# Attention with hashed buckets and two gated layers: sign sums in two PSUM banks, turning of the next pair moved behind other work

## What is computed

```python
# q, k, v: (2, 8, 768, 64)  proj: (64, 6)
q_bits = (einsum('bhsd,dk->bhsk', q, proj) > 0)          # 6 signs per row
k_bits = (einsum('bhsd,dk->bhsk', k, proj) > 0)
mask = (q_bucket[..., :, None] == k_bucket[..., None, :])  # buckets: the 6 signs read as a number
scores = where(mask, scale * q @ k.T, -1e9)
attn = exp(scores - max); attn /= sum(attn) + 1e-9
x = attn @ v                       # (1536, 512) after the heads are joined
x = (sigmoid(x @ w_gate) * (x @ w_val)) @ w_out            # 512 -> 1536 -> 512
h = x @ w_in; x = hinge(h) @ w_out2                        # 512 -> 2048 -> 512
```

## Time and profile before

| | us |
|---|---|
| median of 3 runs | 788.66 (788.01 to 789.24) |
| the profiled execution | 787.32 |
| its span | 785.2 |
| PE busy in the span | 772.7 (98%) |
| DVE, ACT, POOL busy | 557.0, 461.1, 539.0 |

### The profile page before, as it was taken

How to read it: one execution, slowest core, us unless ns; L and a number is a source line. 1 busy time by engine, 2 the same in 40 slices (tenths; PEclk the granted TensorE clock), 3 DMA queues, 4 the chain that set the end, 5 groups by cost and what they waited for, 6 DMA issues and landing times.

```text
span 785.2 us, 12182 instructions
## 1 busy us (share of the span) xinstructions
PE 772.7 (98%) x4403; PEld 716.2 (91%) x4403; DVE 557.0 (71%) x862; ACT 461.1 (59%) x731; POOL 539.0 (69%) x533
## 2 busy tenths in 40 slices
PE   7999999999999999999999999999999999999998
PEld 6999999999989999999899999999899988999996
DVE  6888888888888656565864666676777676756654
ACT  4888988988997443344453333357455465644433
POOL 4667667788889987877596977746957755565420
PEclk9999999999999999999999999999999999999999
DMA  6896586385100222122021211120121111201002
GB/s 153 182 194 135 133 176 132 80 168 131 55 1 1 81 81 81 31 77 81 28 82 55 81 54 53 55 81 28 59 77 55 36 45 45 91 27 54 1 1 80
DMA packets 61930, 60.08 MB, mean 77 GB/s; under 512 B 28384, under 2 KB 51632, under 8 KB 61872
## 3 DMA queue, kind: packets, MB, share of 16 engines
q1 hardware_dynamic: 61712, 59.32, 29.5%
q10 hardware_dynamic: 160, 0.00, 0.0%
HBM read 37.75 MB, written 3.15 MB: 52 GB/s over the span
## 4 chain that ended last, share of the span: by engine, by line
PE 81%; ACT 6%; DVE 5%; issue 4%; POOL 3%; DMA 0%; SPq 0%; POOLq 0%; DVEq 0%; ACTq 0%
PE ps L758 12%; PE ps L759 12%; PE ps L760 12%; PE ps L787 9%; PE ps L799 6%; PE ps L800 6%; PE ps L798 5%; PE ps L788 4%; PE ps L724 4%; ACT ph L916 3%; PE ps L741 2%; PE ps L742 2%; DVE probs L1209 2%; PE ps L712 2%; PE ps L715 2%
## 5 line engine op out<-in xcount | busy, mean ns | idle before, releaser
L758 PE MATMUL ps<-xop,wset 128*128 128x384 f32 x560 | 190.7, 341 | 1.6 <-DVE u L1284 1.4
L759 PE MATMUL ps<-xop,wset 128*128 128x384 f32 x560 | 189.2, 338 | 0.0
L760 PE MATMUL ps<-xop,wset 128*128 128x384 f32 x560 | 188.8, 337 | 0.0
L1284 DVE TENSOR_TENSOR u<-ps,u 128x384 f32<-128x384 f32 x144 | 79.5, 552 | 103.4 <-PE ps L760 102.8
L526 POOL TENSOR_TENSOR wset<-stage,wset 128x512 fp32r<-128x512 f32 x39 | 58.1, 1490 | 108.5 <-ACT wset L963 108.5
L758 PEld LDWEIGHTS ps<-xop,wset 128*128 128x128 f32 x560 | 105.1, 188 | 14.4 <-issue 2.8
L1220 DVE TENSOR_TENSOR pl<-ps,ph 128x768 fp32r<-128x768 f32 x96 | 91.4, 954 | 26.6 <-ACT ph L916 25.7
L759 PEld LDWEIGHTS ps<-xop,wset 128*128 128x128 f32 x560 | 105.3, 188 | 3.5
L501 POOL TENSOR_SCALAR probs<-probs,small 128x768 f32<-128x768 f32 x96 | 88.3, 927 | 24.9 <-DVE small L1214 22.1
L760 PEld LDWEIGHTS ps<-xop,wset 128*128 128x128 f32 x560 | 105.2, 188 | 0.0
L532 POOL TENSOR_TENSOR wset<-wsum,wset 128x1024 fp32r<-128x1024 f32 x39 | 95.2, 2442 | 0.0
(11 more groups left out here) (134 smaller groups left out, 1685.8 us busy)
## 6 DMA issues: line engine op xcount, KB each, us to landing
stage<-in_moe_w_in_dram SPq DMA_DIRECT2D x16, 512.0 KB, 3.4
stage<-in_moe_w_out_dram SPq DMA_DIRECT2D x14, 512.0 KB, 3.8
stage<-in_moe_w_gate_dram SPq DMA_DIRECT2D x12, 512.0 KB, 4.2
stage<-in_moe_w_val_dram SPq DMA_DIRECT2D x12, 512.0 KB, 3.6
ops<-qh SPq DMA_DIRECT2D x15, 384.0 KB, 5.2
ops<-kh SPq DMA_DIRECT2D x28, 192.0 KB, 5.2
qn<-in_q_dram SPq DMA_DIRECT2D x16, 192.0 KB, 4.4
kn<-in_k_dram SPq DMA_DIRECT2D x16, 192.0 KB, 5.3
```

The costliest lines, as they stand in the source:

```text
L758: pe.matmul(dst, high[:, c, :], high_x(r)[:, c, :], start=(c == 0), stop=False)
L759: pe.matmul(dst, high[:, c, :], low_x(r)[:, c, :], start=False, stop=False)
L760: last = pe.matmul(dst, low[:, c, :], high_x(r)[:, c, :], start=False, stop=(c == 1))
```

## The change

The sign sums of q and k of the next pair go to two banks: of q to bank 7, of k to bank 6 (in pair 0's own sums both stay in bank 7). Each is a closed group of six matmuls with its own signal, and each has its own bits, made by an instruction of 64 rows instead of one of 128 for both. The signs of k wait for one more `o_copied`, and the weighings that take bank 7 and bank 6 next wait for the bits of q and of k. All pairs have one timetable: q turned at u = 1 and k at u = 4, signs at u = 3 and u = 6, bits ahead of `evacuate` at u = 4 and u = 7. On TensorE `turn` stands behind the weighing of its step, not ahead of it, and on ScalarE `high_turned` stands behind `exponential`, not ahead of it. The list `uses` follows: Q now stands behind the S and T of u = 1, K behind those of u = 4.

```diff
-        def late(i):
-            return 0 if i else 2
+        TURN = {"Q": 1, "K": 4}
+        SIGNS = {"Q": 3, "K": 6}
+        BITS = {"Q": 4, "K": 7}
...
-            if late(g // U) <= g % U < late(g // U) + 2 and g // U < NP - 1:
-                uses.append(("QK"[g % U - late(g // U)], g // U + 1))
+            for kind in "QK":
+                if g % U == TURN[kind] and g // U < NP - 1:
+                    uses.append((kind, g // U + 1))
...
-        z_bank = ps[:, 7, 0:G]
+        def z_bank(i, keys):
+            return ps[:, 6 if keys and i else 7, 0:G]
+        def bits_made(i, keys):
+            return 2 * i + keys if i else 1
...
-                if u == late(i) + 5 and i < NP - 1:
+                if u == BITS["K"] and i < NP - 1:
                     scale_codes(i + 1)
...
-                if i > 1 and not keys:
-                    pe.wait_ge(o_copied, 4 * (i - 1) - 2)
+                if i > 1:
+                    pe.wait_ge(o_copied, 4 * (i - 1) - (2 - keys))
...
-                        pe.wait_ge(z_bits, 2)
-                    if j % 4 == 3:
-                        pe.wait_ge(z_bits, min((j + 1) // 4 + 2, NP))
+                        pe.wait_ge(z_bits, bits_made(1, False))
+                    if j % 4 == 3 and j // 4 + 2 < NP:
+                        pe.wait_ge(z_bits, bits_made(j // 4 + 2, False))
+                    if j % 4 == 0 and j // 4 + 1 < NP:
+                        pe.wait_ge(z_bits, bits_made(j // 4 + 1, True))
...
-                if u == late(i) and i < NP - 1:
-                    turn("Q", i + 1)
-                if u == late(i) + 1 and i < NP - 1:
-                    turn("K", i + 1)
                 j, part = divmod(g - 8, HT)
                 if j >= 0:
                     weigh(j, part)
-                if u == late(i) + 3 and i < NP - 1:
+                if u == TURN["Q"] and i < NP - 1:
+                    turn("Q", i + 1)
+                if u == TURN["K"] and i < NP - 1:
+                    turn("K", i + 1)
+                if u == SIGNS["Q"] and i < NP - 1:
                     signs(i + 1, False)
-                if u == late(i) + 4 and i < NP - 1:
+                if u == SIGNS["K"] and i < NP - 1:
                     signs(i + 1, True)
...
-                if u == late(i) and i < NP - 1:
+                exponential(g)
+                if u == TURN["Q"] and i < NP - 1:
                     high_turned("Q", i + 1)
-                if u == late(i) + 1 and i < NP - 1:
+                if u == TURN["K"] and i < NP - 1:
                     high_turned("K", i + 1)
-                exponential(g)
...
-                if u == late(i) + 5 and i < NP - 1:
-                    make_bits(i + 1)
+                if u == BITS["Q"] and i < NP - 1:
+                    make_bits(i + 1, False)
+                if u == BITS["K"] and i < NP - 1:
+                    make_bits(i + 1, True)
                 evacuate(g)
```

## The result

The changed kernel takes 796.59 us (795.37 to 799.92, four runs) against 788.61: 1.0107 times as long, interval 1.0091 to 1.0122. The forecast was 795.5, slower. The profiled execution took 795.37 us against 787.32.

A forecast was written before the change was run, and what follows sets the result against it. TensorE was taken to bound the kernel. Pair 0 (+3.2 us) and pairs 1 to 6 (+3.6) gave 6.8 on 787.3, 794.1; the median lies 1.3 above, so 795.5, with an 8-in-10 range of 791 to 799.5.

The forecast's parts named there:

- What bounds the kernel: TensorE, nearly always busy in attention and layers, so attention's gain or loss moves the end one for one.
- Two banks: Second bits instruction on VectorE, 0.6 us in each of seven pairs, hidden behind TensorE; freeing the bank sooner wins nothing: 0.
- the walk: Step-by-step start times for pair 3 and pair 0, built from measured distances between instructions; pair 3 becomes 0.6 us longer.
- Removed stalls: Waits of q at u = 0 and k at u = 1 go: 0.7 us in each of six pairs.
- The new stalls: Scores of u = 3 and 6 wait for low parts of q and k: +3.6 us over pairs 1 to 6.
- the bounds 0 to 1.0: Extra time per steady pair: even if step-to-step edges are 0.1 us shorter, 1.0 us if ScalarE lags more.
- its sign: What the trace after should show: a pair of 29.4 to 29.9 us where it was 29.03.
- Pair 0: First pair, where `evacuate` of u = 2 now stands behind the low part of q: +3.2 us, between +2.0 and +3.6.
- SP's queue: Copies of k and the codes are issued later but still land in time for the next pair: 0.
- the stalls only trade places: Rival: edges are shorter, steady pairs stay even and only pair 0 loses: 791 us, chance 0.13.
- The faster one: Rival: 0.7 us gained in seven pairs because VectorE and ScalarE are never late: 784 us, chance 0.08.
- The growing lag: Rival: ScalarE enters u = 1 later by 0.3 or 0.4 us, 1.0 us or more per pair: 798 to 800, chance 0.12.

The follow-up runs named there:

- e3: The kernel before with two banks alone, turning at its old steps and in its old order: 787.90 us, ratio 0.9998.
- e10: e6 with q's bits of pair 0 at u = 7, not 6: 786.53 us, ratio 0.9982 to the kernel before.
- e5: The changed kernel with idle transposes filling TensorE's idle time in pair 0: 795.80 us, ratio 1.0099 to the kernel before.
- e8: The changed kernel with the second copy of a finished half head ahead of the exponential at u = 2 and 5: 794.03 us.
- e2: The changed kernel with turning ahead of the weighing and high part ahead of the exponential again, timetable and banks kept: 786.59 us, ratio 0.9980.
- e7: The changed kernel with turning ahead of the weighing again, the high part still behind the exponential: 796.18 us, ratio 1.0106 to the kernel before.
- e1: The changed kernel with the high part ahead of the exponential again, turning still behind the weighing: 793.97 us, ratio 1.0067 to the kernel before.
- e9: e1 with the second copy of a finished half head ahead of the exponential at u = 2 and 5: 791.61 us, ratio 1.0046.
- e6: e2 with the old steps of turning, signs and bits in pair 0: 786.26 us, ratio 0.9976 to the kernel before.

## Why the prediction was right
The forecast was 795.5 with 6.8 us of loss; 8.05 us were measured on the profiled executions (787.32 to 795.37) and 8.0 on the medians. In the trace pair 0 lost 3.4 us where 3.2 was said and pairs 1 to 6 lost 5.4 where 3.6 was said; the last pair, which has nothing to turn and no term in the forecast, gained 0.5. So nearly all of the miss is in the steady pairs, and the last pair made good 0.5 us of it by luck.

- *What bounds the kernel.* Right: the layers start 8.4 us later and end 8.4 us later.
- *Two banks.* Forecast 0, e3 measured 0.9998. That VectorE's second bits instruction lies in TensorE's shadow is right for the later pairs; in pair 0 it costs 0.8 us (e10), which the walk of pair 0 had among its steps. The bits of 64 rows take 0.60 to 0.62 us, the whole price of 128 rows, as taken.
- *Removed stalls.* Right: steps 0 and 1 at 2.07 and 2.63 us.
- *The new stalls.* The mechanism was right link by link. Forecast for the scores of u = 3, 4, 6 and 7 of pair 3, counted from the pair's start: 7.36, 10.71, 15.66 and 19.0 us; measured 7.21, 10.72, 15.85 and 19.41. So q's part was right to 0.15 us, k's was too small by 0.4. Two links were left out of the walk. At u = 4 ScalarE makes the high part of the turned probabilities ahead of the exponential, so that the exponential starts at 111.43 and not at 111.07, 0.99 us behind `evacuate` (110.08). And the signs of k do wait for the copy, by 0.18 us, where I had found the two even. The pair is 0.9 us longer, within the bounds 0 to 1.0 but not 0.6, and at 29.96 just above the 29.4 to 29.9 that were named as its sign. The six pairs took 179.5 us and 174.1 before, 5.4 longer, within 0 to +6.
- *Pair 0.* Forecast +3.2, measured +3.4. The walk gave 20.9, 21.6, 22.6, 23.5, 24.35 and 25.4 for bits, `evacuate`, exponential, high part, low part and scores; the rows have 20.86, 21.48, 22.48, 23.42, 24.24 and 25.35. That these agree although TensorE's clock fell beside them, which no term had, is luck: e5 shows that it cost 0.07 us here, e8 that it can cost more.
- *The last pair.* No term. It takes 25.5 us from its u = 0 to its u = 11 and 26.0 before. Before, VectorE's reciprocal at 212.41 waits 0.58 us for GpSimd and step 2 takes 2.58 us; after, that step takes 2.17. What freed GpSimd was not followed further.
- *SP's queue.* Right: no scores of pairs 1 to 6 waited for a DMA. The codes were issued 1.5 us later in the pair than in the walk (from 120.54 to 126.97 us, 22.1 and not 20.6 behind the pair's start), and the next pair's scores still started at 128.41 without a gap.
- *The rivals.* That the stalls only trade places came out in no kernel with the orders of the change. The faster one needed the chain 0.6 us shorter; e2 is the kernel in which this happens, and there the timetable does win, 0.20% or 1.5 us (the rival's own sum should read 4.9 us, seven times 0.7, not 4.7; e2 shows that only half of each 0.7 goes). The growing lag was not seen: after has stalls of 0.1 us at u = 8 and 11, like before.

## What to carry to other kernels
When slots go round between producers, the order of an evacuating engine's queue is part of the ring: a piece of work put ahead of the evacuation costs time as soon as the slot is wanted soon after. Here 0.93 us of exponential and 0.78 us of weighing, twice in a pair, made the pair 1.2 us longer (28.78 to 29.96). Undoing the two orders turned 1.0107 into 0.998, so look at what stands between the fill and the release of a slot on each engine before moving either. Two orders that feed the same instruction do not add: moving the turning alone gave nothing (e7), moving the high part alone 2.6 us (e1), and both together 10 us. And before two profiled executions are compared stage by stage, look in each for waits that have nothing to do with the edit: e1 and e9 have the same order in pair 0 and differ there by 1.3 us, through a wait for a DMA. e6, at 0.9976 (0.9966 to 0.9986), is the fastest kernel found, not clearly ahead of e2.

## What the runs showed of the hardware
TensorE's granted clock can fall inside a kernel that is 98% busy: behind 1.6 to 1.8 us of idle in pair 0 it was 0.65 over 20 to 24 us in the change and 0.76 in e2, and 1.00 with the idle filled (e5). Idle time alone does not decide it: in e1's profiled execution TensorE stood idle 2.44 us at the same place and the clock stayed at 1.00, and in e8's it fell only behind a second idle, of 1.91 us, and then to 0.50. What it costs depends on what TensorE is waiting for: nothing in the change (25.79 against 25.72 us with the idle filled), some 2.5 us in the profiled execution of e8 (an estimate: pair 0 took 28.27 there, against 25.79). An instruction of VectorE over 64 rows took 0.60 to 0.62 us, the same as the 0.62 over 128 rows.
